# Another order of the transfers in the second MoE of a fused attention and two-MoE kernel

## The reference

```python
def _moe_ref(x, w_in, w_out):            # x: 4608 x 512, w_in: 512 x 2048, w_out: 2048 x 512
    h = x @ w_in
    g = h - np.tanh(h)
    return g @ w_out

def _moe2_ref(x, w_in, w_out, s, b):     # the same sizes
    h = x @ w_in
    r = np.maximum(h, 0.0)
    g = s * (r * r) + b
    return g @ w_out
```

## Time and profile before

| | us |
|---|---|
| median of 3 runs | 1466.71 (1465.81 to 1467.6) |
| the profiled execution, its own time | 1464.37 |
| its span in the profile | 1462.6 |
| mean granted TensorE clock, share of full | 0.999 |
| TensorE busy | 1450.0 (99%) |
| VectorE busy | 869.6 (59%) |
| ScalarE busy | 580.2 (40%) |
| DMA queue of SP, share of 16 engines' span | 42.6% |

### The profile page before, as it was taken

The page is one execution under the profiler, slowest core; times in us unless marked ns, Lnnn a source line. Parts: engine busy times, 40 slices in busy tenths (PEclk is TensorE's granted clock), DMA queues, the critical chain, the costliest instruction groups (busy, mean ns, idle before and its releaser), DMA issues.

```text
span 1462.6 us, 24312 instructions
## 1 busy us (share of the span) xinstructions
PE 1450.0 (99%) x9838; PEld 1272.7 (87%) x9838; DVE 869.6 (59%) x1582; ACT 580.2 (40%) x1116; POOL 80.5 (6%) x71
## 2 busy tenths in 40 slices
PE   8999999999999999999999999999999999999999
PEld 6989989999998989999988888788887888888887
DVE  6755655656555565567767545854566545854563
ACT  3444344444444444445534322732145322732243
POOL 3700101001010010000000000000000000000000
PEclk9999999999999999999999999999999999999999
DMA  9402322122222212032494554846466554846235
GB/s 351 166 5 82 114 82 63 68 82 100 82 84 96 72 60 71 18 103 87 190 386 148 217 208 158 320 155 253 172 226 249 211 213 158 323 155 252 69 120 197
DMA packets 79679, 225.45 MB, mean 154 GB/s; under 512 B 5584, under 2 KB 34384, under 8 KB 74960
## 3 DMA queue, kind: packets, MB, share of 16 engines
q1 hardware_dynamic: 79568, 223.89, 42.6%
HBM read 181.93 MB, written 41.94 MB: 153 GB/s over the span
## 4 chain that ended last, share of the span: by engine, by line
PE 95%; DMA 4%; DVE 1%; issue 0%; SPq 0%; ACT 0%; DVEq 0%
PE banks L240 31%; PE banks L241 30%; PE banks L242 30%; DMA w_out_ring<-w_out_parts_scratch 3%; PE banks L548 2%; PE banks L495 1%; PE banks L517 1%; PE banks L565 1%; PE banks L503 0%; DMA kT<-k_T 0%; PE banks L485 0%; PE banks L526 0%; PE banks L504 0%; DVE m_parts L1009 0%; DVE probs L1018 0%
## 5 line engine op out<-in xcount | busy, mean ns | idle before, releaser
L240 PE MATMUL banks<-g_high,w_out_parts 128*128 128x288 f32 x1024 | 309.9, 303 | 0.0
L242 PE MATMUL banks<-g_high,w_out_parts 128*128 128x288 f32 x1024 | 301.6, 295 | 0.0
L241 PE MATMUL banks<-g_low,w_out_parts 128*128 128x288 f32 x1024 | 301.4, 294 | 0.0
L1173 DVE TENSOR_TENSOR g<-banks,g 128x288 f32<-128x288 f32 x256 | 117.0, 457 | 198.0 <-ACT g L833 196.5
L240 PE MATMUL banks<-g_high,w_out_ring 128*128 128x512 f32 x576 | 225.3, 391 | 5.6 <-DMA w_out_ring<-w_out_parts_scratch 5.6
L884 ACT ACTIVATE g<-g,small 128x512 f32<-128x512 f32 x144 | 117.3, 815 | 285.8 <-DVE g L1259 284.6
L240 PEld LDWEIGHTS banks<-g_high,w_out_parts 128*128 128x128 f32 x1024 | 192.0, 187 | 38.8 <-issue 32.1
L241 PE MATMUL banks<-g_low,w_out_ring 128*128 128x512 f32 x576 | 224.7, 390 | 0.0
L242 PE MATMUL banks<-g_high,w_out_ring 128*128 128x512 f32 x576 | 224.6, 390 | 0.0
L833 ACT ACTIVATE g<-banks 128x288 f32<-128x288 f32 x256 | 105.4, 412 | 273.8 <-PE banks L242 272.7
L242 PEld LDWEIGHTS banks<-g_high,w_out_parts 128*128 128x128 f32 x1024 | 192.3, 188 | 0.0
(11 more groups left out here) (155 smaller groups left out, 1989.1 us busy)
## 6 DMA issues: line engine op xcount, KB each, us to landing
w_out_ring<-w_out_parts_scratch SPq DMA_DIRECT2D x144, 512.0 KB, 4.6
w_in_first<-w_in_operands_scratch SPq DMA_DIRECT2D x28, 1792.0 KB, 7.5
kT<-k_T SPq DMA_DIRECT2D x16, 576.0 KB, 4.1
qT<-q_T SPq DMA_DIRECT2D x16, 576.0 KB, 6.3
x1T_scratch<-x_store SPq DMA_DIRECT2D x16, 576.0 KB, 3.8
v_rows<-v_rows SPq DMA_DIRECT2D x8, 1024.0 KB, 5.6
w_out_parts_scratch<-w_out_stage SPq DMA_DIRECT2D x16, 512.0 KB, 2.7
out_T<-y_store SPq DMA_DIRECT2D x8, 1024.0 KB, 7.5
```

What stands on the lines that cost most here:

```text
L240: nc.tensor.matmul(out, high, rhigh, start=first, stop=False)
L241: nc.tensor.matmul(out, high, rlow, start=False, stop=False)
L242: return nc.tensor.matmul(out, low, rhigh, start=False, stop=last)
L1173: nc.vector.tensor_tensor(TG1[:, c % 2, :], HB[:, c % 2, 0:U1], TG1[:, c % 2, :], ALU.subtract).then_inc(g_done, 1)
```

## The change

In round 0 the two chunk loads of a step come first, then one operand's store, in the order 0, 1, 2, 4, 5, 6, 7, 3, one in each step (before, 0 and 1 in step 0, 2 and 3 in step 1, then 4, 5, 6, 7). The four x blocks, which were loaded together in step 1 ahead of its chunks, are loaded two in step 1 and two in step 2, behind the chunks and the store. In a turn, the x blocks of the next round, two ahead of chunk load b - 2 and two ahead of chunk load b, come one behind each of the chunk loads b - 2 to b + 1. The store of y moves from behind chunk load b + 2 to behind b + 4, and the load of the operand for buffer 3 from behind b + 3 to behind b + 13. No transfer is added, removed or resized.

```diff
             for q in range(PF):
-                for f in {0: (0, 1), 1: (2, 3), 2: (4,), 3: (5,), 4: (6,), 5: (7,)}.get(q, ()):
-                    store_w_in2(f)
-                if q == 1:
-                    sp.wait_ge(xo_ready, NPR)
-                    for i in range(4):
-                        load_x_block(1, i)
                 if q >= 1:
                     next_w_out2(2 * q - 2)
                     next_w_out2(2 * q - 1)
+
+                store_w_in2((0, 1, 2, 4, 5, 6, 7, 3)[q])
+                if q == 1:
+                    sp.wait_ge(xo_ready, NPR)
+                for i in {1: (0, 3), 2: (2, 1)}.get(q, ()):
+                    load_x_block(1, i)
...
                 for i in range(-2, FC - 2):
-                    if n < WIDE and i == -2:
+                    next_w_out2(b + i)
+                    if n < WIDE and i < 2:
                         sp.wait_ge(prod_done, NPR * PF * (n + 1))
-                        load_x_block(n + 1, 0)
-                        load_x_block(n + 1, 3)
-                    if n < WIDE and i == 0:
-                        load_x_block(n + 1, 2)
-                        load_x_block(n + 1, 1)
-                    next_w_out2(b + i)
-                    if i == 2:
+                        load_x_block(n + 1, (0, 3, 2, 1)[i + 2])
+                    if i == 4:
                         store_y(2 * n - 1)
-                    if i == 3:
-                        next_w_in2(n, PF - 1)
+                next_w_in2(n, PF - 1)
```

## The result

The changed kernel has a median of 1456.52 us (1456.46 to 1456.66, four executions) beside 1467.15 (1465.81 to 1468.39) for the kernel before: a ratio of 0.9928, with a 95% interval of 0.9911 to 0.9945, or 10.6 us. I had forecast 1459.3, in a range from 1457.3 to 1463.0. The direction is right, the time lies 0.8 us outside the range, and the gain is 1.4 times the 7.4 us of the sum.

The account below looks back on a forecast made before the run. TensorE bounds the kernel, stalling on w_out2 chunks late behind queued bytes. Removing 8.1 us, less 0.7 for later x blocks, took the profiled 1464.37 to 1457.0; 2.3 us up to the median gave 1459.3, range 1457.3 to 1463.

Parts of the forecast that it names:

- the sum: Whole kernel: 8.1 us of stall and clock loss removed, less 0.7 for later x blocks, a gain of 7.4 us.
- Bound and place of the stalls: TensorE waits four times for w_out2 chunks, in round 0 and three turns, 5.6 us, behind queued bytes.
- The clock: Round 0, behind the stall: TensorE at 1.2 GHz from 748.0 to 751.4, losing 1.6 us; no such stretch in the turns.
- The stall's idle time in round 0: TensorE's wait at 745.5 us for the first chunk, 2.46 us long.
- The turns: Three turns between rounds: waits of 1.35 and 1.8 us plus restart losses, 3.9 us gained before the x blocks' cost.
- Cost of chunks in round 0: Two chunks, an operand and blocks drain in 9.3 us of each 10.5 us step, so chunks cost nothing.
- Store 5: Round 0, moved behind chunk load 7: lands in 7.5 to 9.4 us, cost 0; at 11.7 it costs 2.1.
- store 7: Round 0, issued at 782.7: lands by 792.1, ACT wants it at 790.4, needed only at 799.6, cost 0.
- Cost of the later x blocks: Turns: DVE waits 1.8 to 2.1 us for block 3; cost 0.2 us a turn, 0.7 in all, at most 4.
- the sign of being wrong there: Turns: the prediction is wrong if TensorE waits over 0.5 us for the low part of g.
- Bandwidth: The skill page's 358 GB/s against the trace's 425; by the page the turns would lose some 2 us more.
- Rivals: Three: covers break in part, 1461.7 to 1464.7 (0.17); another engine holds the gain, 1463.5 (0.05); late block drops clock, 1471 (0.03).

Follow-up runs that it names:

- e8_fill: Kernel before, transfers untouched, with 12 float32 matmuls of zeros filling TensorE's stall in round 0: 1465.0 us, ratio 0.9983.
- e4_wait_late: Kernel before, with only SP's wait for the stores of x moved from ahead of the operand stores to behind them: 1464.63 us, ratio 0.9984.
- e0_before: Kernel before, run again with no edit: median 1467.52 us over 12 executions.
- e1_round0: Kernel before with only the round 0 part of the change, turns as before: 1461.15 us, ratio 0.9965.
- e2_turns: Kernel before with only the turns part of the change, round 0 as before: 1461.68 us, ratio 0.9969.
- e6: Changed kernel with the x blocks of the turns back in pairs at their old places: 1456.20 us over four executions.
- e11: Changed kernel with the x blocks of the turns back in pairs at their old places, run a second time: 1456.16 us over five executions.

## Why the prediction was wrong in size

**The step that failed** is the last one of the sum: "It lies 2.3 us below the median of 1466.71, so I forecast a median of 1459.3 us." That treated the distance between the profiled execution and the median as something that the change leaves alone. It is made, for the most part, of what the change removes: the terms that I read from that one execution, 4.3 us for round 0 and 3.9 for the turns, are too small. In the runs of the halves round 0 is 5.1 to 5.8, and the turns are 4.5 to 5.3 where I had 3.2 after the cost; that is 2.1 to 3.6 us more, and the forecast missed by 2.8. Every other profile with the old order shows a longer stall in round 0 or longer waits in the turns. Against the profiled execution itself the sum was near: 1464.37 - 8.1 + 0.7 of cost gave 1457.0, with no cost 1456.3, and measured was 1456.46. In the runs of the result the kernel without these stalls shows no such distance (median 1456.52, profile 1456.46, spread 0.2 us). In the next job it has a spread of 2 us and a profiled execution 1.6 above the median, with the 1.9 us lost ahead of round 0, so a part of any such distance is outside the change. Before, the spread was 2.6 us in the first runs shown and 8 over 72 executions. That three executions spread by 1.8 us and the profile lay outside them was in the table; I used it only as noise of the range.

Point by point:
- *Bound and place of the stalls*: right. Both kinds are gone, and each half of the change alone removes its own.
- *The clock*: right in kind, 1.6 us in the first profile; in a median execution 2.6 (`e8_fill`), and 2.9 and 2.4 in two more profiles, whose stretch at 1.2 GHz was 6.6 us. That the shorter stalls of the turns cost no clock was true of the first profile, not of every execution: in `e4_wait_late` one of 1.93 us did, 1.7 us.
- *The stall's idle time in round 0*: 2.46 us was a short one; 2.99 and 4.69 in two more profiles. One cause is borne out: the wait for the last store of x, 3.6 to 5.5 us ahead of the stores, as far as the DMA engines stand idle in it. It is not the only one: `e0_before` began its stores 0.14 us earlier than the first profile and stalled 0.5 us longer.
- *The turns*: 3.9 us less the 0.7 of the blocks, so 3.2; 4.5 to 5.3 measured (`e1_round0`, `e2_turns`). The 1.8 and 1.35 us of idle time were those of an execution with short waits.
- *Cost of chunks in round 0*: 0, right; the first landed in 3.1 us. Store 5 landed in 8.0 us, inside my 7.5 to 9.4, and L1132 did not wait. ScalarE waited 1.6 us for store 7, where I had 1.7, and nothing waited for it.
- *Cost of the later x blocks*: VectorE waited 1.5 and 0.6 us in the turn of round 1, since block 3 landed in 4.6 us. I had 1.8 to 2.1 for the first and about 2 for the second, and the second was wrong: it landed 3.1 us behind the first (921.11 + 5.0 against 918.38 + 4.6), and VectorE works for 2.4 us from one `mix_x` to the next, so only 0.6 were left. TensorE's weight loads waited 0.4 us at most in a turn and 0.6 over all three, about the 0.5 that I had set as the sign of being wrong there; it cost no more than I had charged. I charged 0.7; `e6` and `e11` put it at 0.4.
- *Bandwidth*: the 358 GB/s of the Trainium skill, *DMA: Bandwidth & Descriptors*, section Bandwidth, did not bear here either: the windows of the changed kernel beside 748 us have 408 and 397. I had read the page too narrowly. The same section gives that figure for two cores that both stream from one memory domain, and one core runs here.
- *Rivals*: none came. All of mine made the gain smaller; none asked whether the profiled execution stood for the others.

Still open: why the last store of x takes 3.6 us in one execution and 5.5 in another, why the same order of transfers stalled the turn of round 1 by 1.35 to 2.62 us, what makes the clock fall at 15 to 25 us in some executions, and how much of the 8 us spread belongs to each.

## What to carry to other kernels

Terms read from one profiled execution give the difference to that execution. Before adding the sum to the median, ask of what the distance between the two is made: a stall on queued bytes, and a clock that falls on it, differ from execution to execution, and a change that removes them removes that part of the distance too. In one queue with a ring of loads that are due on time, put what is due first ahead and the bulk behind it, and put the bulk where no load is due for longer than the bulk takes; moving a smaller transfer without the bulky one can make it worse.

## What the runs showed of the hardware

With the same order of transfers, the stretch at 1.2 GHz was about 3.4 us behind a stall of 2.46 us and 6.6 us around one of 2.99. A stall of 1.93 us in the turn of round 2 (`e4_wait_late`) had a stretch of some 3.4 us as well, while one of 2.62 us in the turn of round 1 (`e1_round0`) and one of 0.82 left the clock at 1.00. So the length of a stall alone did not decide it here.

Float32 matmuls of zeros in the stall kept it at 1.00; in the profile the chunk came 0.33 us after they ended, so there they cost nothing.

A wait of the issuing engine cost the queue only what the DMA engines did not move meanwhile. With 288 GB/s still moving, a start 3.7 us earlier brought a chunk behind 9.4 MB only 1.7 us forward, at the same 382 and 385 GB/s on the way; with 15 GB/s for the last 2 us, a start 2.05 us later made the stall 2.2 us longer.
